# Two heads of q and k transposed side by side, and stacked by copies inside SBUF

## The chip, the cores and the metric

The kernel runs on one core of a Trainium2 chip. The metric is the device time of one execution in microseconds (us).

## What is computed

The reference runs attention over 8 batches and 8 heads of 576 positions by 64 dimensions, with all scores that lie more than tau under their row's maximum dropped, then two mixing layers. Only the attention is touched here:

```python
scores = scale * np.matmul(q, k.transpose(0, 1, 3, 2))
thresh = np.max(scores, axis=-1, keepdims=True) - tau
scores = np.where(scores >= thresh, scores, -1000000000.0)
scores = scores - np.max(scores, axis=-1, keepdims=True)
attn = np.exp(scores)
attn = attn / (np.sum(attn, axis=-1, keepdims=True) + 1e-09)
return np.matmul(attn, v).astype(np.float32)
```

## The kernel before

The attention walks over 32 pairs of heads. The 2 x 576 query rows of a pair are nine tiles of 128 rows: tiles 0 to 7 take the first 512 rows of the two heads in turn, tile 8 the last 64 rows of both. Every engine has its own list of steps for a pair, written out by hand: `PE_PLAN`, `ACT_PLAN` and `DVE_PLAN`. A step's name is its kind and number, and a trailing minus marks a step that belongs to the pair before. `scores` is the product q k^T of a tile in two halves of 288 keys (L434), `max` and `mask` are VectorE's row maximum (L561) and threshold product (L566), `exp` is ScalarE's small threshold operation and its exponential (L504, L506), `probs` and `rem` are transposes of the result (L395) with ScalarE's copy out of PSUM (L487), `pv` is the product with v (L476). `k`, `q` and `kq` prepare the next pair: transposes of its keys, its queries and its last 64 rows, with ScalarE's copies (L487, L491).

PSUM has three slots for scores, so tile i + 3 waits for the mask of tile i, and two banks `aux_ps` that all transposes and the product with v take in turn. So a group on TensorE waits until ScalarE has copied the group two before it.

The products are made in two passes of a rounded type: k is parted into k_hi and k_lo and q into a high and a low part, and one matmul multiplies the stack [q_hi; q_lo] on 128 partitions with [k; k], each head's 64 rows twice. Before, the doubling of k is done by the loads: `k_nat` holds each row twice side by side, so that its transpose has it on both halves of the partitions. q is parted in its natural layout by GpSimd (`q_split`, L318 and L320) and the two parts are transposed together. A pair thus takes 8 transposes for k, 8 for q and 2 for the last rows. After ScalarE's copy GpSimd parts k (`split_k`, L331 to L337). The first pair's k is parted by VectorE (L581 to L587).

SyncE (SP) issues the DMAs in the order of its `run`: `spread` (the reciprocal row sums to DRAM, L253 and L255, a wait for their landing, and their broadcast back, L258), the loads of q and k for the pair after the next (L202, L206, L235, L237), v, a chunk of weights (L241), and the store of x (L247). Between the runs of pairs 0 and 1 it issues seven small loads of the mixing's vectors (L289). ScalarE issues four large copies of weights from DRAM to DRAM, one after each of the exponentials 0 to 3 of pair 0 (L510). GpSimd's `run` also parts the chunk of weights (L343, L345) and multiplies x by the reciprocals (L358, L361).

## Time and profile before

| what | value |
|---|---|
| median of 3 runs | 1361.78 us (1361.44 to 1362.06) |
| the profiled execution, its own time | 1362.08 us |
| its span | 1360.3 us |
| busy TensorE, VectorE, ScalarE, GpSimd | 1325.3, 893.7, 876.1, 322.5 us |
| attention | from the start to about 629 us |

The span is what the trace covers; the time has 1.8 us more around it. Start times in the rows below count from the span's start. PE is TensorE's matmuls and PEld its weight loads, of which each matmul has one; PEld's starts are the better clock for TensorE's pace, since the ends of matmuls are modelled. DVE is VectorE, ACT ScalarE, POOL GpSimd, SPq SyncE's DMA queue. A bracket at the end of a row is idle time of the engine before it and what ended it.

### The profile page before, as it was taken

Reading aid. Unit: us, or ns where it says so; the run is one execution under the profiler, and the core shown is the slowest. Engines: PE = TensorE matmul, PEld = TensorE weight load, DVE = VectorE, ACT = ScalarE, POOL = GpSimd, SP = SyncE. Lnnn points to the kernel's source line nnn. Section 1 sums busy time; section 2 is a strip of 40 time slices with the busy share of each in tenths; the row PEclk is TensorE's granted clock in tenths of the full one; section 3 lists DMA queues with packets and bytes.
Section 4 is the critical chain, followed back from the end, with each engine's and each line's share of the span. In section 5 each row is a group of like instructions: output and inputs, shape, how many; then the busy total and the mean of one; then the engine's idle time right before and its main releaser. Section 6 shows DMA issues by size and latency. Waiting matters only on the chain.

```text
span 1360.3 us, 30705 instructions
## 1 busy us (share of the span) xinstructions
PE 1325.3 (97%) x9628; PEld 1161.0 (85%) x9628; DVE 893.7 (66%) x1969; ACT 876.1 (64%) x2086; POOL 322.5 (24%) x433
## 2 busy tenths in 40 slices
PE   6999999999999999996999999999999999999998
PEld 5777777777777777774999999999999999999997
DVE  4777777777777777775766765576647665756544
ACT  5888888888888888884545544554445445534432
POOL 3455554455544555533000000000000000000000
PEclk8999999999999999997999999999999999999999
DMA  8534433334333344322010011001110111011000
GB/s 234 131 101 113 116 94 105 104 103 116 101 103 104 99 115 116 93 77 87 19 34 17 18 34 42 19 18 34 34 40 5 34 34 34 1 42 34 17 9 32
DMA packets 141082, 90.49 MB, mean 67 GB/s; under 512 B 96192, under 2 KB 125120, under 8 KB 140992
## 3 DMA queue, kind: packets, MB, share of 16 engines
q1 hardware_dynamic: 137360, 82.47, 21.6%
q10 hardware_dynamic: 3632, 6.88, 1.5%
q8 instruction: 49, 0.80, 0.3%
q14 instruction: 41, 0.34, 0.1%
HBM read 70.29 MB, written 25.31 MB: 70 GB/s over the span
## 4 chain that ended last, share of the span: by engine, by line
PE 52%; DVE 1%; ACT 0%; issue 0%; DVEq 0%
PE kv_ps L805 15%; PE kv_ps L886 15%; PE vr_ps L805 15%; PE y_ps L870 7%; DVE mixed L998 0%; DVE xm_lo L1004 0%; ACT mixed L918 0%; DVE x L1057 0%; ACT xm_hi L926 0%; ACT y L935 0%; DVE square L1015 0%; DVE g_lo L1030 0%; DVE x_lo L1062 0%; DVE gated L1025 0%; ACT g_hi L966 0%
## 5 line engine op out<-in xcount | busy, mean ns | idle before, releaser
L566 DVE SCALAR_TENSOR_TENSOR probs<-score_ps,threshold,probs 128x576 f32<-128x576 f32 x288 | 234.5, 816 | 72.2 <-ACT probs L506 70.4
L561 DVE TENSOR_REDUCE neg_max<-score_ps 128x1 f32<-128x576 f32 x288 | 209.8, 747 | 95.6 <-PE score_ps L434 93.3
L506 ACT ACTIVATE probs<-score_ps,neg_max 128x576 f32<-128x576 f32 x288 | 215.3, 747 | 0.0
L487 ACT ACTIVATE probsT<-aux_ps 128x512 f32<-128x512 f32 x288 | 168.2, 615 | 44.3 <-PE aux_ps L395 44.3
L395 PE MATMUL aux_ps<-ident,probs 128*128 128x128 f32 x1280 | 190.5, 279 | 3.9 <-ACT k_raw L487 2.6
L434 PE MATMUL score_ps<-k_lo,qT 128*128 128x288 f32 x512 | 166.5, 340 | 5.0 <-DVE probs L566 4.2
L805 PE MATMUL kv_ps<-xm_hi,w_lo 128*128 128x288 f32 x512 | 152.5, 298 | 13.9 <-DVE xm_lo L1004 11.1
L395 PEld LDWEIGHTS aux_ps<-ident,probs 128*128 128x128 f32 x1280 | 144.5, 141 | 24.8 <-ACT probsT L487 10.9
L805 PE MATMUL kv_ps<-xm_hi,w_hi 128*128 128x288 f32 x512 | 152.5, 298 | 0.0
L805 PE MATMUL kv_ps<-xm_lo,w_hi 128*128 128x288 f32 x512 | 152.3, 297 | 0.0
L886 PE MATMUL kv_ps<-kk_hi,w_hi 128*128 128x288 f32 x512 | 151.1, 295 | 0.0
L886 PE MATMUL kv_ps<-kk_lo,w_hi 128*128 128x288 f32 x512 | 150.9, 295 | 0.0
L886 PE MATMUL kv_ps<-kk_hi,w_lo 128*128 128x288 f32 x512 | 150.2, 293 | 0.0
L434 PE MATMUL score_ps<-k_hi,qT 128*128 128x288 f32 x512 | 144.5, 297 | 0.0
L1070 DVE SCALAR_TENSOR_TENSOR gate<-x,taps,gate 128x288 f32<-128x288 f32 x256 | 132.2, 516 | 18.7 <-ACT gate L955 15.3
L476 PE MATMUL aux_ps<-probsT,v_nat 128*64 128x320 f32 (+1 forms) x1024 | 138.3, 412 | 1.0 <-ACT probsT_rem L487 0.8
L795 POOL MEMSET x_in<- 128x4 f32 x7 | 0.7, 105 | 545.1 <-DVE mixed L998 545.1
L434 PEld LDWEIGHTS score_ps<-k_lo,qT 128*128 128x128 f32 x512 | 97.1, 190 | 21.3 <-issue 14.6
L805 PEld LDWEIGHTS kv_ps<-xm_hi,w_lo 128*128 128x128 f32 x512 | 97.6, 191 | 16.0 <-DVE xm_lo L1004 12.7
L476 PEld LDWEIGHTS aux_ps<-probsT,v_nat 128*64 128x64 f32 x1024 | 68.2, 136 | 49.8 <-issue 10.8
L955 ACT ACTIVATE gate<-x,taps 128x288 f32<-128x288 f32 x64 | 34.1, 533 | 115.4 <-DVE x L1057 115.4
L945 ACT ACTIVATE relu<-kv_ps 128x288 f32<-128x288 f32 x128 | 52.3, 409 | 86.0 <-PE kv_ps L805 83.6
(99 smaller groups left out, 3216.7 us busy)
## 6 DMA issues: line engine op xcount, KB each, us to landing
k_nat<-in_k SPq DMA_DIRECT2D x128, 128.0 KB, 2.5
recip_rows<-recip_scratch SPq DMA_DIRECT2D x64, 144.0 KB, 3.1
x_scratch<-x_out SPq DMA_DIRECT2D x32, 288.0 KB, 2.6
out<-y SPq DMA_DIRECT2D x36, 256.0 KB, 2.0
q_nat<-in_q SPq DMA_DIRECT2D x31, 256.0 KB, 2.8
v_nat<-in_v SPq DMA_DIRECT2D x31, 256.0 KB, 2.7
w_stage<-packed SPq DMA_DIRECT2D x32, 192.0 KB, 2.5
x_in<-x_scratch SPq DMA_DIRECT2D x8, 578.0 KB, 4.1
```

The costliest lines, as they stand in the source:

```text
L395: return nc.tensor.transpose(out, in_, ident[:])
L434: last = nc.tensor.matmul(score_ps[i % SLOTS][:, half, 0:HALF], w, m, start=(term == 0), stop=(term == len(parts) - 1))
L476: last = nc.tensor.matmul(bank[D * h:D * (h + 1), 0:cols.stop - cols.start], v_nat[rows, cc % 2, h * FULL + t if t < FULL else MIX, :], m, ...
L487: return nc.scalar.activation(out, in_, ACT.Copy)
L506: nc.scalar.activation(tile_halves(i), scored(i), ACT.Exp, bias=neg_max[:, i:i + 1], scale=1.0).then_inc(exp_done, 1)
L561: nc.vector.tensor_reduce(neg_max[:, i:i + 1], scored(i), mybir.AxisListType.XY, ALU.max, negate=True).then_inc(max_ready, 1)
L566: nc.vector.scalar_tensor_tensor(tile_halves(i), scored(i), threshold[:, i:i + 1], tile_halves(i), ALU.is_ge, ALU.mult, accum_out=row_sum[ ...
L805: last = nc.tensor.matmul(ps, w, m, start=(n == 0), stop=(n == 3 * len(terms) - 1))
L870: last = nc.tensor.matmul(y_ps[i % 2][:], g[:, ch, col:col + P], w[:, ch, :], start=(n == 0), stop=(n == 3 * C - 1))
L886: last = nc.tensor.matmul(kv_ps[u][:, 0:HT], w, m[:, j, :], start=(n == 0), stop=(n == 3 * CF - 1))
L945: nc.scalar.activation(relu[:, i % 2, :], kv_ps[i % 4][:, 0:HT], ACT.Relu).then_inc(relu_done, 1)
L1070: nc.vector.scalar_tensor_tensor(gate[:, u, :], x2[:, u, t:t + HT], taps[:, t, u:u + 1], gate[:, u, :], ALU.mult, ALU.add).then_inc(conv_s ...
```

## The change

q and k of the pair's two heads are loaded side by side in the columns of `qk_nat`, each once, so that one transpose of 128 by 128 gives head 0 on partitions 0 to 63 and head 1 on 64 to 127. The last rows of q and k lie in `rem_nat` and take one transpose. A pair has 4 + 4 + 1 transposes in three groups in place of 18 in five. ScalarE copies the results to `q_raw` and `k_raw`. GpSimd now parts both after the transposes: `split_k` as two rounding copies and two subtractions over 640 and 576 columns, and after it `split_q` as two rounding copies and one subtraction over 640 columns. Each part then lies on the wrong half of the partitions for one of its uses, and SyncE copies it over within SBUF: `stack_k` waits for the whole of `split_k` and issues four DMAs of 64 partitions by 576 or 640 columns, `stack_q` waits for `split_q` and issues two of 64 by 640. TensorE's `scores0` of a pair waits for all six.

In the plans the preparing steps of the next pair are moved from the end of a pair to its start, and `exp8`, `max8`, `mask8` and `probs3` from the next pair to the end of their own. In SyncE's `run` the loads of q and k come first, then `stack_k`, `spread`, `stack_q` and the rest. In GpSimd's `run` the two splits come ahead of the weights' chunk. At the start SyncE stacks pair 0 as well, and the 12 warming matmuls of 512 columns are 14 of 128 columns in another type. The diff's core:

```diff
--- before.py
+++ after.py
 PE_PLAN = steps("""
-    scores0 probs3- probs7- scores1 pv0- scores2 probs6- probs8- scores3 q0 rem1- scores4
-    probs0 pv1- kq0 scores5 k0 rem0 scores6 probs2 k1 scores7 probs1 q1 scores8 probs4 probs5
+    scores0 k0 q0 scores1 probs7- probs6- scores2 kq0 pv0- probs8- scores3 probs0 rem1- scores4
+    scores5 pv1- scores6 probs3 probs4 scores7 rem0 probs2 scores8 probs5 probs1
 """)
 ACT_PLAN = steps("""
-    probs3- exp8- probs7- exp0 exp1 pv0- probs6- probs8- q0 rem1- probs0 exp2 exp3 exp4 pv1-
-    kq0 k0 rem0 exp5 probs2 k1 exp6 probs1 q1 exp7 probs4 probs5
+    k0 q0 probs7- probs6- exp0 kq0 exp1 exp2 pv0- probs8- probs0 rem1- exp3 exp4 exp5 pv1-
+    probs3 probs4 exp6 rem0 probs2 exp7 probs5 probs1 exp8
 """)
 DVE_PLAN = steps("""
-    max8- max0 max1 mask8- mask0 mask1 recip0- max2 max4 max3 mask2 mask3 max5 mask4 max6
-    mask5 max7 mask6 mask7
+    max0 recip0- max1 max2 mask0 mask1 mask2 max3 max4 max5 mask3 mask4 max6 mask5 max7 mask6
+    max8 mask7 mask8
 """)
-FIRST_PREPARE = steps("k0 kq0 k1 q0 q1")
+FIRST_PREPARE = steps("k0 kq0 q0")
...
-        q_nat = sb("q_nat", [P, 2, TILES, D])
-        k_nat = sb("k_nat", [P, 2, TILES, 2, D])
+        qk_nat = sb("qk_nat", [P, 2, 2, FULL, 2 * D])
+        rem_nat = sb("rem_nat", [P, 2, 2 * D])
         v_nat = sb("v_nat", [P, 2, TILES, D])
-        q_split = sb("q_split", [P, TILES, 2, D])
-        qT = sb("qT", [P, 2, 2, MAIN], F32R)
-        q_rem = sb("q_rem", [P, 2, 4, REM], F32R)
-        k_raw = sb("k_raw", [P, 2 * S])
-        k_hi = sb("k_hi", [P, 2, 2 * S + REM], F32R)
-        k_lo = sb("k_lo", [P, 2, 2 * S + REM], F32R)
+        q_raw = sb("q_raw", [P, QW])
+        k_raw = sb("k_raw", [P, KW])
+        q_lo = sb("q_lo", [P, QW], F32R)
+        q_all = sb("q_all", [P, 2, 2 * QW + REM], F32R)
+        k_hi = sb("k_hi", [P, 2, S + KW], F32R)
+        k_lo = sb("k_lo", [P, 2, S + KW], F32R)
...
+        def load_qk(eng, n, name, it, c, loaded):
+            for h in range(2):
+                eng.dma_start(qk_nat[:, c % 2, n, :, h * D:(h + 1) * D],
+                              heads[name][it * 4 + (2 * c + h), 0:MAIN, :].rearrange(
+                                  "(p t) d -> p t d", t=FULL)).then_inc(loaded[c % 2], 16)
+            eng.dma_start(rem_nat[n * REM:(n + 1) * REM, c % 2, :].rearrange("p (h d) -> p h d", h=2),
+                          heads[name][bass.ds(it * 4 + 2 * c, 2), MAIN:S, :].rearrange(
+                              "h p d -> p h d")).then_inc(loaded[c % 2], 16)
...
-                def load_k(it, c):
-                    slot = c % 2
-                    for twice in range(2):
-                        for h in range(2):
-                            head = it * 4 + (2 * c + h)
-                            k_to = k_nat[:, slot, :, twice, :]
-                            sp.dma_start(k_to[:, h * FULL:(h + 1) * FULL, :], heads["k"][head, 0:MAIN, :].rearrange(
-                                "(p t) d -> p t d", t=FULL)).then_inc(k_loaded[slot], 16)
-                            sp.dma_start(k_to[REM * h:REM * (h + 1), MIX, :],
-                                         heads["k"][head, MAIN:S, :]).then_inc(k_loaded[slot], 16)
+                def stack_q(it, c):
+                    par = c % 2
+                    sp.wait_ge(q_steps, count(it, c, 3, 3))
+                    sp.dma_start(q_all[REM:P, par, 0:QW].bitcast(F32), q_lo[0:REM, :].bitcast(F32)).then_inc(q_stacked, 16)
+                    sp.dma_start(q_all[0:REM, par, H1:].bitcast(F32), q_lo[REM:P, :].bitcast(F32)).then_inc(q_stacked, 16)
+                def stack_k(it, c):
+                    sp.wait_ge(k_steps, count(it, c, 4, 4))
+                    for kk in (k_lo, k_hi):
+                        own = kk[:, c % 2, :].bitcast(F32)
+                        sp.dma_start(own[REM:P, 0:S], own[0:REM, 0:S]).then_inc(k_stacked, 16)
+                        sp.dma_start(own[0:REM, S:], own[REM:P, S:]).then_inc(k_stacked, 16)
...
                 def run(it, c):
+                    if c <= PAIRS - 3:
+                        sp.wait_ge(aux_full, turns(it, prepared(c - 1)))
+                        load_q(sp, it, c + 2)
+                        load_k(sp, it, c + 2)
+                    if c < PAIRS - 1:
+                        stack_k(it, c + 1)
                     if c > 0:
                         spread(it, c - 1)
-                    if c <= PAIRS - 3:
-                        sp.wait_ge(aux_full, turns(it, prepared(c - 1)))
-                        load_q(sp, it, c + 2)
-                        load_k(it, c + 2)
                     if c < PAIRS - 1:
+                        stack_q(it, c + 1)
                         if c > 0:
                             sp.wait_ge(aux_full, turns(it, number_of(c - 1, "pv", 1) + 1))
                         load_v(sp, it, c + 1)
...
-                load_k(0, 0)
+                load_k(sp, 0, 0)
                 load_q(sp, 0, 1)
-                load_k(0, 1)
+                load_k(sp, 0, 1)
+                stack_k(0, 0)
+                stack_q(0, 0)
                 run(0, 0)
...
-                def split_q(it, c):
-                    wait(q_loaded[c % 2], count_loaded(it, c, 3))
-                    nc.gpsimd.tensor_copy(q_split[:, :, 0, :].bitcast(F32R), q_nat[:, c % 2, :, :]).then_inc(q_steps, 1)
-                    wait(q_steps, count(it, c, 2, 1))
-                    nc.gpsimd.tensor_tensor(q_split[:, :, 1, :], q_nat[:, c % 2, :, :], q_split[:, :, 0, :],
+                def split_q(it, c, run):
+                    wait(aux_copied, turns(it, 1 + max(number(run, (x, 0, False)) for x in ("q", "kq"))))
+                    for at in (0, H1):
+                        nc.gpsimd.tensor_copy(q_all[:, c % 2, at:at + QW], q_raw[:]).then_inc(q_steps, 1)
+                    wait(q_steps, count(it, c, 3, 1))
+                    nc.gpsimd.tensor_tensor(q_lo[:], q_raw[:], q_all[:, c % 2, 0:QW].bitcast(F32),
                                             ALU.subtract).then_inc(q_steps, 1)
                 def split_k(it, c, run):
-                    for h in range(2):
-                        ready = max(number(run, ("k", h, False)), number(run, ("kq", 0, False)))
-                        wait(aux_copied, turns(it, ready + 1))
-                        to = slice(h * S, (h + 1) * S)
-                        hi, lo = k_hi[:, c % 2, :], k_lo[:, c % 2, :]
-                        if h == 1:
-                            nc.gpsimd.tensor_copy(hi[:, 2 * S:], k_raw[:, S:S + REM])
-                        nc.gpsimd.tensor_copy(hi[:, to], k_raw[:, to]).then_inc(k_steps, 1)
-                        wait(k_steps, count(it, c, 4, 2 * h + 1))
-                        if h == 1:
-                            nc.gpsimd.tensor_tensor(lo[:, 2 * S:], k_raw[:, S:S + REM], hi[:, 2 * S:].bitcast(F32),
-                                                    ALU.subtract)
-                        nc.gpsimd.tensor_tensor(lo[:, to], k_raw[:, to], hi[:, to].bitcast(F32),
+                    wait(aux_copied, turns(it, 1 + max(number(run, (x, 0, False)) for x in ("k", "kq"))))
+                    parts = ((slice(S, S + KW), k_raw[:]), (slice(0, S), k_raw[:, REM:]))
+                    for to, raw in parts:
+                        nc.gpsimd.tensor_copy(k_hi[:, c % 2, to], raw).then_inc(k_steps, 1)
+                    wait(k_steps, count(it, c, 4, 2))
+                    for to, raw in parts:
+                        nc.gpsimd.tensor_tensor(k_lo[:, c % 2, to], raw, k_hi[:, c % 2, to].bitcast(F32),
                                                 ALU.subtract).then_inc(k_steps, 1)
...
                 def run(it, c):
                     if c > 0:
                         sums(it, c - 1)
-                        split_w(it, c - 1)
                     if c < PAIRS - 1:
                         split_k(it, c + 1, c)
+                        split_q(it, c + 1, c)
                     if c > 0:
+                        split_w(it, c - 1)
                         normalize(it, c - 1)
-                    if c < PAIRS - 2:
-                        wait(aux_full, turns(it, prepared(c)))
-                        split_q(it, c + 2)
-                split_q(0, 0)
-                pool.wait_ge(aux_full, prepared(-1))
-                split_q(0, 1)
+                split_q(0, 0, -1)
...
-                pe.wait_ge(ident_made, 2)
-                for _ in range(12):
-                    nc.tensor.matmul(aux_ps[0][:], q_rem[:, 0, 0:2, :], q_rem[:], start=True, stop=True)
                 pe.wait_ge(ident_made, 3)
...
                             if i == 0:
-                                pe.wait_ge(aux_copied, turns(it, prepared(c - 1)))
-                                pe.wait_ge(k_steps, count(it, c, 4, 2))
-                            if i == 1:
-                                pe.wait_ge(k_steps, count(it, c, 4, 4))
+                                pe.wait_ge(q_stacked, count(it, c, 32, 32))
+                                pe.wait_ge(k_stacked, count(it, c, 64, 64))
...
                         elif kind == "k":
-                            pe.wait_ge(k_loaded[(c + 1) % 2], count_loaded(it, c + 1, 8))
+                            pe.wait_ge(k_loaded[(c + 1) % 2], count_loaded(it, c + 1, 3))
                             for t in range(FULL):
-                                last = transpose(blocks[:, t, :], k_nat[:, (c + 1) % 2, i * FULL + t, :, :])
+                                last = transpose(blocks[:, t, :], qk_nat[:, (c + 1) % 2, 1, t, :])
                         elif kind == "q":
-                            pe.wait_ge(q_steps, count(it, c + 1, 2, 2))
+                            pe.wait_ge(q_loaded[(c + 1) % 2], count_loaded(it, c + 1, 3))
                             for t in range(FULL):
-                                last = transpose(blocks[:, t, :], q_split[:, i * FULL + t, :, :])
+                                last = transpose(blocks[:, t, :], qk_nat[:, (c + 1) % 2, 0, t, :])
                         elif kind == "kq":
-                            pe.wait_ge(k_loaded[(c + 1) % 2], count_loaded(it, c + 1, 8))
-                            pe.wait_ge(q_steps, count(it, c + 1, 2, 2))
-                            transpose(blocks[:, 0, :], q_split[:, MIX, :, :])
-                            last = transpose(blocks[:, 1, :], k_nat[:, (c + 1) % 2, MIX, :, :])
+                            pe.wait_ge(k_loaded[(c + 1) % 2], count_loaded(it, c + 1, 3))
+                            pe.wait_ge(q_loaded[(c + 1) % 2], count_loaded(it, c + 1, 3))
+                            last = transpose(blocks[:, 0, :], rem_nat[:, (c + 1) % 2, :])
...
+                for _ in range(14):
+                    nc.tensor.matmul(aux_ps[0][:, 0:P], ident[:], ident[:], start=True, stop=True)
...
                         elif kind == "q":
-                            scale_q(qT[:, nxt, i, :], bank[:]).then_inc(aux_copied, 1)
+                            scale_q(q_raw[:, 2 * REM:], bank[:]).then_inc(aux_copied, 1)
                         elif kind == "k":
-                            copy(k_raw[:, i * (S + REM):i * (S + REM) + MAIN], bank[:]).then_inc(aux_copied, 1)
+                            copy(k_raw[:, REM:S], bank[:]).then_inc(aux_copied, 1)
                         elif kind == "kq":
-                            scale_q(q_rem[:, nxt, 0:4:3, :], blocks[:, 0, :].rearrange("p (h q) -> p h q", h=2))
-                            copy(k_raw[:, MAIN:S + REM], blocks[:, 1, :]).then_inc(aux_copied, 1)
+                            scale_q(q_raw[:, 0:REM], bank[:, 0:REM])
+                            copy(k_raw[:].rearrange("p (a b) -> p a b", b=REM)[:, 0:TILES + 1:TILES, :],
+                                 bank[:, REM:2 * REM].unsqueeze(1).broadcast_to([P, 2, REM])).then_inc(aux_copied, 1)
```

## Rows read from the trace of the kernel before

**Rows 1.** Windows: busy us and instructions of each engine, granted clock, DMA share, GB/s.

```profile
200.00:300.00 100.00, 99.84 (x766) 76.30 (x764) 72.79 (x150) 88.42 (x204) 55.09 (x73) 1.00 0.40 107
```

**Rows 2.** Timeline, PEld: first weight load of scores0 of pair 2 and of pair 31.

```profile
51.64 0.19 PEld L434 LDWEIGHTS score_ps<-k_lo,qT 128*128 128x128 f32 x1
...
594.52 0.19 PEld L434 LDWEIGHTS score_ps<-k_lo,qT 128*128 128x128 f32 x1
```

**Rows 3.** Timeline, PEld: a scores step, a group of four transposes, what follows.

```profile
269.99 0.19 PEld L434 LDWEIGHTS score_ps<-k_lo,qT 128*128 128x128 f32 x1
...
270.51 0.49 PEld L395 LDWEIGHTS aux_ps<-ident,k_nat 128*128 128x128 f32 x4
270.97 0.25 PEld L395 LDWEIGHTS aux_ps<-ident,probs 128*128 128x128 f32 x2
```

**Rows 4.** Timeline, ScalarE, in a steady pair.

```profile
270.30 0.37 ACT L491 ACTIVATE q_rem<-aux_ps,q_scale 128x128 fp32r<-128x128 f32 x1
270.57 0.27 ACT L487 ACTIVATE k_raw<-aux_ps 128x128 f32<-128x128 f32 x1
271.28 0.60 ACT L487 ACTIVATE k_raw<-aux_ps 128x512 f32<-128x512 f32 x1 [0.45 <-PE aux_ps L395]
...
273.80 0.32 ACT L504 ACTIVATE threshold<-neg_max,tau_down 128x1 f32<-128x1 f32 x1
...
274.60 0.63 ACT L487 ACTIVATE probsT<-aux_ps 128x512 f32<-128x512 f32 x1
275.08 0.73 ACT L491 ACTIVATE qT<-aux_ps,q_scale 128x512 fp32r<-128x512 f32 x1
```

**Rows 5.** Timeline, GpSimd: the first head's k is parted.

```profile
272.01 0.66 POOL L332 CAST k_hi<-k_raw 128x576 fp32r<-128x576 f32 x1 [6.60 <-ACT k_raw L487]
272.82 1.43 POOL L337 TENSOR_TENSOR k_lo<-k_raw,k_hi 128x576 fp32r<-128x576 f32 x1
```

**Rows 6.** Timeline, SyncE's DMA issues: spread, then loads.

```profile
266.27 0.70 SPq L253 DMA_DIRECT2D recip_scratch<-recip_T  x1
267.01 0.62 SPq L255 DMA_DIRECT2D recip_scratch<-recip_T  x1
268.65 1.14 SPq L258 DMA_DIRECT2D recip_rows<-recip_scratch  x2
270.07 0.40 SPq L202 DMA_DIRECT2D q_nat<-in_q  x1
...
273.42 0.58 SPq L235 DMA_DIRECT2D k_nat<-in_k  x1
274.10 0.57 SPq L237 DMA_DIRECT2D k_nat<-in_k  x1
```

**Rows 7.** DMA view, 100 to 500 us: KB of each, median us from issue to landing.

```profile
recip_rows<-recip_scratch SPq DMA_DIRECT2D x44, 144.0 KB, 3.1
x_scratch<-x_out SPq DMA_DIRECT2D x21, 288.0 KB, 2.6
```

**Rows 8.** DMA view, whole span.

```profile
out<-y SPq DMA_DIRECT2D x36, 256.0 KB, 2.0
```

**Rows 9.** DMA view, 14 to 45 us: loads beside the copies of weights.

```profile
k_nat<-in_k SPq DMA_DIRECT2D x4, 128.0 KB, 12.0
```

**Rows 10.** Timeline, the start: q_scale, the first split, pair 0's first scores.

```profile
7.10 0.14 DVE L553 TENSOR_SCALAR q_scale<-tau_sb 128x1 f32<-128x1 f32 x1
10.76 0.46 DVE L582 CAST k_hi<-k_raw 128x576 fp32r<-128x576 f32 x1 [3.52 <-ACT k_raw L487]
11.26 0.76 DVE L587 TENSOR_TENSOR k_lo<-k_raw,k_hi 128x576 fp32r<-128x576 f32 x1
...
14.01 0.40 PE L434 MATMUL score_ps<-k_lo,qT 128*128 128x288 f32 x1 [0.78 <-ACT qT L491]
```

**Rows 11.** Timeline, SyncE: first of the small loads, and the first issue behind them.

```profile
28.27 0.69 SPq L289 DMA_DIRECT2D mu<-in_moe_mu_k  x1
...
42.61 0.75 SPq L253 DMA_DIRECT2D recip_scratch<-recip_T  x1
```

More of the change, by code:

```diff
@@ L261, in run @@
                 def run(it, c):
-                    if c > 0:
-                        spread(it, c - 1)
                     if c <= PAIRS - 3:
@@ L395, in transpose, with query @@
                     return nc.tensor.transpose(out, in_, ident[:])
+                def query(h, i, par):
+                    at = h * (H1 - REM) + (0 if i == MIX else (2 + h) * REM + i // 2 * P)
+                    return q_all[:, par, at:at + P]
                 def transpose_mixed(out, in_):
@@ L415, in run @@
                             if i == 0:
-                                pe.wait_ge(aux_copied, turns(it, prepared(c - 1)))
-                                pe.wait_ge(k_steps, count(it, c, 4, 2))
-                            if i == 1:
-                                pe.wait_ge(k_steps, count(it, c, 4, 4))
+                                pe.wait_ge(q_stacked, count(it, c, 32, 32))
+                                pe.wait_ge(k_stacked, count(it, c, 64, 64))
                             if c > 0 or i >= SLOTS:
                                 pe.wait_ge(probs_ready, count(it, c, TILES, i + 1 - SLOTS))
+                            ps = score_ps[i % SLOTS]
+                            parts = (i % 2,) if i < MIX else (0, 1)
                             for half in range(2):
-                                def keys(kk, at):
-                                    return kk[:, par, at + half * HALF:at + (half + 1) * HALF]
-                                if i < MIX:
-                                    h, t = i % 2, i // 2
-                                    parts = [(qT[:, par, h, t * P:(t + 1) * P], keys(kk, h * S)) for kk in (k_lo, k_hi)]
-                                else:
-                                    parts = [(q_rem[:, par, 2 * h:2 * h + 2, :], keys(kk, h * (S + REM)))
-                                             for kk in (k_lo, k_hi) for h in range(2)]
-                                for term, (w, m) in enumerate(parts):
-                                    last = nc.tensor.matmul(score_ps[i % SLOTS][:, half, 0:HALF], w, m,
-                                                            start=(term == 0), stop=(term == len(parts) - 1))
+                                terms = [(kk, h) for kk in (k_lo, k_hi) for h in parts]
+                                for n, (kk, h) in enumerate(terms):
+                                    at = S * h + (REM if h and i == MIX else 0) + half * HALF
+                                    last = nc.tensor.matmul(ps[:, half, 0:HALF], query(h, i, par), kk[:, par, at:at + HALF],
+                                                            start=(n == 0), stop=(n == len(terms) - 1))
                             last.then_inc(scores_full, 1)
@@ L572, in run @@
                             nc.vector.reciprocal(recip[:], row_sum[:, cc % 2, :]).then_inc(recip_ready, 1)
[L574 to L587 removed]
+                dve.wait_ge(aux_copied, 1 + max(number(-1, (x, 0, False)) for x in ("k", "kq")))
+                parts = ((slice(S, S + KW), k_raw[:]), (slice(0, S), k_raw[:, REM:]))
+                for to, raw in parts:
+                    nc.vector.tensor_copy(k_hi[:, 0, to], raw).then_inc(k_steps, 1)
+                dve.wait_ge(k_steps, 2)
+                for to, raw in parts:
+                    nc.vector.tensor_tensor(k_lo[:, 0, to], raw, k_hi[:, 0, to].bitcast(F32),
                                             ALU.subtract).then_inc(k_steps, 1)
```

31 lines of the change are left out of this document (13 added, 18 removed).

## The prediction, made before the changed kernel was seen to run

> **What bounds the kernel now.** I read the windows view first. In the middle of the attention TensorE is busy for 99.84 of 100 us, ScalarE for 88.42, VectorE for 72.79 and GpSimd for 55.09, at a granted clock of 1.00 [rows 1]. The reader should see an engine with no room beside one with little. Next the pace: scores0 of pair 2 starts at 51.64 and that of pair 31 at 594.52, so a pair takes 542.88 / 29 = 18.72 us [rows 2]. Weight loads show what a step costs on TensorE: a scores step of four matmuls runs from 269.99 to 270.51, 0.52 us, and four transposes from 270.51 to 270.97, 0.46 us, so 0.115 each [rows 3]. TensorE's order of work bounds the attention, with short waits for the two banks that ScalarE empties. The mixing after it is untouched.
>
> **What is removed.** Nine of 18 transposes of a pair: 9 x 0.115 = 1.04 us of TensorE, 1.0 rounded down. ScalarE loses one copy for k and one for q, starts 0.48 and some 0.58 apart (a copy of 512 columns starts at 274.60 and the next step at 275.08; the scaling one lasts 0.10 longer) [rows 4]: 1.06 us. Both bounds thus fall by the same amount, and a pair bound as before would take 18.72 - 1.0 = 17.7 us. Over 29 pairs that is 29 us. VectorE's work per pair is the same. k's loads fall from eight DMAs to three, and q's stay at three.
>
> **What is added: a loop through four engines.** The old stacking cost nothing after GpSimd. Now scores0 of the next pair waits for k and q of that pair to be transposed, copied, parted and stacked, and these steps only begin behind scores0 of this pair. What is queued behind the wait on TensorE is the whole next pair, its preparing transposes included, so a late stack delays its own successor and the loop's length becomes the pace. I add it up from scores0 at 0, with ScalarE free, as it is if TensorE has waited.
>
> - TensorE: scores0 to 0.52, k0 to 0.98. ScalarE starts a copy 0.77 after the first of four transposes (270.51 to 271.28) [rows 3, 4], so k0's copy is at 1.29 and q0's at 1.77 to 2.35. probs6- needs the bank of q0, so it starts at 2.5 and its copy is at 3.25 to 3.75. exp0 takes 0.80 (273.80 to 274.60), to 4.55, and kq0's two copies about 0.27 each by the old ones of 0.37 and 0.27 at 270.30 and 270.57 [rows 4]. Sum: 5.1 us. (Without a wait before, ScalarE is some 0.35 later.)
> - GpSimd starts 0.13 after the copy's end (271.28 + 0.60 to 272.01) [rows 4, 5]. The casts take 0.66 us for 576 columns and the subtraction 1.43, 0.15 behind the cast [rows 5]. For 640 columns I scale by 1.11: 0.73 and 1.59. split_k is 0.13 + 0.73 + 0.66 + 0.15 + 1.59 + 1.43, less about 0.2 for starts that overlap: 4.5 us. k is ready at 9.6. split_q follows with 0.73 + 0.73 + 1.59, less 0.1: 2.95, at 12.5.
> - SyncE: stack_k issues four DMAs. Issues in a row start 0.74 apart in spread's stores (266.27 and 267.01), 0.67 apart in k's loads, and two broadcasts end 1.14 after the first's start, under 0.6 each. The least duration is 0.40, of one after a pause [rows 6]. No row shows a copy from SBUF to SBUF. I take 0.62 each, since these run back to back, and 0.40 to 0.70 as bounds: 2.5 us (1.6 to 2.8).
> - spread stands between stack_k and stack_q. It runs from 266.27 to the next issue at 270.07, 3.8 us, of which 1.0 is the wait for the two stores to land [rows 6]. Its input is there by then, since rem1- is copied at about 9. The bound below is 3.8, above 4.4 if the stores queue behind 600 KB of stacks.
> - stack_q: its second DMA starts 0.62 later and lands after 2.0 us (256 KB, alone on the queue) [rows 8] to 3.1 (144 KB broadcast from DRAM) [rows 7]. The store of x takes 2.6. The copies are 160 KB and read SBUF in long rows, so I take 2.3, nearest to the 2.0.
>
> The sum is 5.1 + 4.5 + 2.5 + 3.8 + 0.6 + 2.3 = 18.8 us, and with all SyncE terms at their ends 5.1 + 4.5 + 1.6 + 3.8 + 0.4 + 2.0 = 17.4 and 5.1 + 4.5 + 2.8 + 4.4 + 0.7 + 3.1 = 20.6. It is over the 17.7 of TensorE's work. So TensorE waits 1.1 us at every scores0, and the pace is 18.8 in place of 18.72: 29 x 0.08 = +2 us. split_q at 12.5 is not late; SyncE comes to it at 15.9.
>
> The Trainium skill ("DMA: Bandwidth & Descriptors", Anatomy of one DMA) gives a fit of 2.0 us and bytes over 436 GB/s for a DMA on GpSimd's path. By that an estimate for 160 KB is 2.4 us, and the sum above would be 18.9. Its rules for kernel authors say that two transfers to disjoint partition halves aren't worth splitting since they share the same engines, which speaks against halves as the unit here; no row before shows it.
>
> **Once only: the start.** Before, pair 0's scores start at 14.01. ScalarE can't scale before q_scale at 7.24 [rows 10]. From there: k0 and kq0 copied at 8.4, VectorE's parts of k (0.46 and 0.76 for 576 columns [rows 10], twice, the larger ones a tenth more) to 11.1, q's copy at 9.5 and GpSimd's part of it to 12.6, stack_k to 13.6, stack_q's last issue at 14.2, landed at 16.5, scores0 about 16.6: +2.6 us.
>
> Then SyncE's seven small loads cost 42.61 - 28.27 = 14.3 us of issue [rows 11], and they stand ahead of stack_k and stack_q of pair 2. Before, nothing urgent stood behind them. Pair 0's scores at 16.6, kq0 and GpSimd's two splits for pair 1 (5.0 and 7.5) to 29.1, stack_q to 30.3, v and weights 2.5, small loads from 32.8 to 47.1, six loads 3.7, stack_k 2.5, spread 3.8, stack_q and landing 2.9: pair 2's scores0 at 60.0, against 51.64 [rows 2], +8.4 us. Pair 1's stacks fall beside the copies of weights, where a load took 12.0 us to land [rows 9], and SyncE's issues may be held up there as well. That can add up to 4, and I take 1.6, so +10 us in all (6 to 13), the first 2.6 included. If the 14.3 us were not in the way, +3 would be left. The tail has one group of four transposes less: -0.5.
>
> **Sum.** 1362.08 (the profiled execution's own time, 1360.3 of it span) + 10 + 2 - 0.5 = 1373.6, 1373.3 beside the median, which is 0.3 lower. The two one-time terms are rough; I state 1373.
>
> **Rivals.**
> - The stacks are hidden. If an issue costs 0.40 and the landing 2.0, the loop is 17.4, under 17.7; TensorE's work sets the pace, -29 + 9.5 = 1342. For it: the short issues of 0.40 exist [rows 6]. Against: DMAs issued in a row take 0.57 to 0.74 each there. Chance 0.14.
> - The loop binds, but just: issues 0.55, landing 2.0, so 5.1 + 4.5 + 2.2 + 3.8 + 0.55 + 2.0 = 18.15, 29 x -0.57 + 9.5 = 1355. Chance 0.16. It decides at 18.72 - 9.5 / 29 = 18.39 us: shorter loops make the kernel faster, longer ones slower.
> - The loop is longer: spread's stores and the last stacks queue behind the four stacks. Spread 4.3, issues 0.67, landing 2.6 give 5.1 + 4.5 + 2.7 + 4.3 + 0.7 + 2.6 = 19.9, 29 x 1.18 + 9.5 = 1406; half of that excess, 19.35, gives 1390. Chance 0.2 for 19.2 and more.
> - The start costs little (SyncE's small loads go faster away from the copies of weights): pace 18.8, start +3: 1366. Chance 0.08.
>
> **How the numbers follow.** The forecast, loops of 18.4 to 19.2 with the start near +10, has 0.42 and its own range is 1361 to 1385. A measurement of this kernel can tell about 0.2% from no change, 2.7 us. Faster takes the first two rivals, 0.14 and 0.13 of 0.16, and nothing else: 0.27. Within 0.2% takes 0.03 of the second, 0.03 of the last and the forecast's lower edge, 0.07: 0.13. The rest is slower: 0.60. For 8 in 10 I leave out most of the first rival and the far end of the third: 1346 to 1394.
>
> **What the profile would show.** TensorE should have an idle of about 1 us before the first weight load of each pair's scores0, released by a DMA into q_all, and busy under 96% in the window of rows 1. kq0's copies should end about 5.1 behind scores0, GpSimd's k_lo 4.5 later, SyncE's four stacks start 0.6 apart, spread take 3.8, and the last stack land 2.3 after its issue. Pair 2's scores0 should start near 61, with an idle of several us. I am wrong if TensorE has no idle there and a pair takes 17.7, or if ScalarE or VectorE hold the new order up.

## The result and the profile after

The changed kernel takes 1419.5 us (median; 1419.0 to 1423.2) against 1361.9 in the same session: a ratio of 1.043, with an interval of 1.041 to 1.0446. The span went from 1360.3 to 1421.3. The forecast of 1373 and its range up to 1394 are missed on the slow side. The profiled execution of the changed kernel is the slowest of the four, 1423.2 us. Times below are medians; of the run with `spread` ahead of both stacks one execution of four (1409.6 us) fell in a slower state and is left out. The lines below answer to [rows 1] and [rows 2]; the first two are the page's busy times and the windows view (its stretch and length, then busy us and instructions of PE, PEld, DVE, ACT, POOL, then granted clock, DMA share, GB/s).

```profile
PE 1308.0 (92%) x9356; PEld 1154.6 (81%) x9356; DVE 900.4 (63%) x1967; ACT 841.0 (59%) x2022; POOL 338.9 (24%) x404
...
200.00:300.00 100.00, 87.93 (x649) 67.88 (x648) 67.32 (x138) 74.82 (x175) 49.12 (x59) 0.97 0.50 131
```

```profile
17.56 0.28 PEld L449 LDWEIGHTS score_ps<-k_lo,q_all 128*128 128x128 f32 x1 [8.83 <-DMA q_all<-q_lo]
...
62.37 0.19 PEld L449 LDWEIGHTS score_ps<-k_lo,q_all 128*128 128x128 f32 x1 [4.15 <-issue]
...
659.89 0.19 PEld L449 LDWEIGHTS score_ps<-k_lo,q_all 128*128 128x128 f32 x1 [2.19 <-DMA q_all<-q_lo]
```

No engine is full any more: TensorE fell from 99.84 to 87.93 busy, and ScalarE, VectorE and GpSimd fell as well. A pair takes (659.89 - 62.37) / 29 = 20.60 us against 18.72. The waits view of 100 to 500 us names who is waited for (us in all, times, longest; a mean of 38.4 / 17 = 2.3):

```profile
PE score_ps L449 <- DMA q_all<-q_lo: 38.4, 17, 2.9
```

The span's 61.0 us divide so. Pair 2's scores start at 62.37 in place of 51.64: +10.7. Then 29 x 1.88 = +54.6. What is left is -4.4, and it lies in the mixing, from its first matmul to the end: 724.5 us (1421.3 - 696.84) against 728.8 (1360.3 - 631.46). From the last pair's scores0 to that matmul it is 36.95 and 36.94, the same. The mixing's code is untouched. The first 60 weight loads of the mixing take 14.3 us before and 10.0 after, which is all of the difference. These rows, of before and then of after, show what stands beside them:

```profile
631.76 0.61 POOL L787 CAST w_out_hi<-y 128x512 fp32r<-128x512 f32 x1 [2.55 <-DMA y<-in_moe_w_out]
632.60 1.52 DVE L998 SCALAR_TENSOR_TENSOR mixed<-x_in,mu,mixed 128x288 f32<-128x288 f32 x1
634.05 0.86 DVE L1004 TENSOR_TENSOR xm_lo<-mixed,xm_hi 128x288 fp32r<-128x288 f32 x1
634.96 0.29 PEld L805 LDWEIGHTS kv_ps<-xm_hi,w_lo 128*128 128x128 f32 x1 [1.49 <-DVE xm_lo L1004]
```

```profile
697.56 0.51 DVE L1008 SCALAR_TENSOR_TENSOR mixed<-x_in,mu,mixed 128x288 f32<-128x288 f32 x1
697.99 0.45 DVE L1014 TENSOR_TENSOR xm_lo<-mixed,xm_hi 128x288 fp32r<-128x288 f32 x1
699.05 0.65 POOL L797 CAST w_out_hi<-y 128x512 fp32r<-128x512 f32 x1 [4.46 <-DMA y<-in_moe_w_out]
```

VectorE's same two operations take 0.51 and 0.45 us while GpSimd is idle, and 1.52 and 0.86 while GpSimd parts w_out. Before, GpSimd begins 0.3 us after the mixing's first matmul (631.76), so TensorE waits for VectorE three times, 3.1 us in all, and its clock is at the lower level for the first 10.4 us; after, GpSimd begins 2.2 us behind it (699.05), those waits are gone, and it is so for 4.4 us. The experiments below bear this out: in the two with fillers GpSimd begins 0.0 and 0.4 us behind, and the mixing takes 729.0 and 729.1 us; in the other seven it begins 1.6 to 2.3 behind, and the mixing takes 724.4 to 725.4. Moving GpSimd's work by itself was not tried.

**One pair, step by step.** The timeline of after, with PEld, ScalarE's last copy (kq0 for k), GpSimd's two splits and SyncE's issues:

```profile
271.39 0.19 PEld L449 LDWEIGHTS score_ps<-k_lo,q_all 128*128 128x128 f32 x1 [2.16 <-issue]
...
276.07 0.28 ACT L503 ACTIVATE k_raw<-aux_ps 128x128 f32<-128x128 f32 x1
...
276.49 1.33 POOL L359 CAST k_hi<-k_raw 128x640 fp32r<-128x640 f32 x2 [4.15 <-ACT k_raw L503]
277.97 2.93 POOL L362 TENSOR_TENSOR k_lo<-k_raw,k_hi 128x640 fp32r<-128x640 f32 x2 [0.15 <-POOL k_hi L359]
...
280.93 0.53 SPq L260 DMA_DIRECT2D k_lo<-k_lo  x1
281.50 0.60 SPq L261 DMA_DIRECT2D k_lo<-k_lo  x1
282.14 0.60 SPq L260 DMA_DIRECT2D k_hi<-k_hi  x1
282.79 0.60 SPq L261 DMA_DIRECT2D k_hi<-k_hi  x1
283.51 0.69 SPq L276 DMA_DIRECT2D recip_scratch<-recip_T  x1
284.24 0.61 SPq L278 DMA_DIRECT2D recip_scratch<-recip_T  x1
285.86 1.14 SPq L281 DMA_DIRECT2D recip_rows<-recip_scratch  x2
287.13 0.51 SPq L252 DMA_DIRECT2D q_all<-q_lo  x1
287.68 0.60 SPq L253 DMA_DIRECT2D q_all<-q_lo  x1
...
291.56 0.25 PEld L449 LDWEIGHTS score_ps<-k_lo,q_all 128*128 128x128 f32 x1 [2.80 <-DVE probs L582]
...
297.81 0.29 ACT L503 ACTIVATE k_raw<-aux_ps 128x128 f32<-128x128 f32 x1
```

Read it as a loop. kq0 is copied 4.96 us after scores0 (276.35). GpSimd ends 4.55 later, SyncE starts 0.03 after that, its issues run for 6.75 to the last one, and scores0 follows 3.88 behind: 20.17 in all. The bracket of the next scores0 names a release by VectorE, but its product for probs was long done. The DMA is what came last.

The last row shows a second thing. In the pair that starts at 291.56, kq0 is copied after 6.54 us. TensorE waits 2.2 to 2.8 us at scores0 (once 3.1), and in every second or third pair the granted clock is at its lower level (1.2 GHz) behind the wait. Eight transposes show it: 0.92 us of weight loads in the one pair, 1.71 in the other.

```profile
271.89 0.92 PEld L412 LDWEIGHTS aux_ps<-ident,qk_nat 128*128 128x128 f32 x8
...
292.45 1.71 PEld L412 LDWEIGHTS aux_ps<-ident,qk_nat 128*128 128x128 f32 x8
```

The DMA view of 100 to 500 us (KB each, median us from issue to landing) has the disputed transfer:

```profile
q_all<-q_lo SPq DMA_DIRECT2D x40, 160.0 KB, 3.3
...
recip_rows<-recip_scratch SPq DMA_DIRECT2D x38, 144.0 KB, 3.1
...
k_hi<-k_hi SPq DMA_DIRECT2D x19, 160.0 KB, 2.6
```

The same 160 KB copy lands in 2.6 us as part of k's stack and in 3.3 as part of q's, behind the two broadcasts. The four stacks of k are themselves issued 0.6 apart, so the later ones have up to three copies of 144 to 160 KB under way ahead of them, and they land no later for it.

**The start.** Pair 1's scores0, and SyncE's small loads:

```profile
39.30 0.29 PEld L449 LDWEIGHTS score_ps<-k_lo,q_all 128*128 128x128 f32 x1 [4.61 <-issue]
...
30.86 0.60 SPq L253 DMA_DIRECT2D q_all<-q_lo  x1
...
34.14 0.53 SPq L317 DMA_DIRECT2D mu<-in_moe_mu_k  x1
...
45.88 1.25 SPq L218 DMA_DIRECT2D qk_nat<-in_q  x2
```

Pair 1 starts 8.4 us behind its last copy's issue (30.86 to 39.30), since that copy, beside ScalarE's copies of weights, takes 8.2 us to land. The small loads hold SyncE from 34.14 to 45.88.

### The profile page after: what moved, and what is told of

It is laid out like the page before. It is cut to its first block, busy times and chain, and to the rows that moved or that the text cites. A ratio compares the mean times of both kernels' runs of the same rounds, so it can differ in the third digit from the quotient of the medians.

```text
span 1421.3 us, 29572 instructions
## 1 busy us (share of the span) xinstructions
PE 1308.0 (92%) x9356; PEld 1154.6 (81%) x9356; DVE 900.4 (63%) x1967; ACT 841.0 (59%) x2022; POOL 338.9 (24%) x404
## 4 chain that ended last, share of the span: by engine, by line
PE 49%; DVE 1%; ACT 0%; issue 0%; DVEq 0%
PE kv_ps L896 14%; PE vr_ps L815 14%; PE kv_ps L815 13%; PE y_ps L880 7%; DVE xm_lo L1014 0%; DVE square L1025 0%; DVE mixed L1008 0%; ACT mixed L928 0%; DVE x L1067 0%; DVE kk_lo L1029 0%; ACT xm_hi L936 0%; ACT y L945 0%; DVE g_lo L1040 0%; DVE x_lo L1072 0%; DVE gated L1035 0%
## 5 line engine op out<-in xcount | busy, mean ns | idle before, releaser
L577 DVE TENSOR_REDUCE neg_max<-score_ps 128x1 f32<-128x576 f32 x288 | 215.0, 756 | 168.9 <-PE score_ps L449 164.9
L449 PE MATMUL score_ps<-k_lo,q_all 128*128 128x288 f32 x640 | 202.9, 346 | 86.6 <-DMA q_all<-q_lo 70.4
L449 PEld LDWEIGHTS score_ps<-k_lo,q_all 128*128 128x128 f32 x640 | 123.7, 200 | 110.0 <-issue 62.5
L503 ACT ACTIVATE probsT<-aux_ps 128x512 f32<-128x512 f32 x288 | 163.7, 604 | 55.6 <-PE aux_ps L412 52.0
L412 PE MATMUL aux_ps<-ident,probs 128*128 128x128 f32 x1280 | 184.1, 280 | 1.0 <-ACT probsT L503 0.8
L449 PE MATMUL score_ps<-k_hi,q_all 128*128 128x288 f32 x640 | 178.7, 307 | 0.0
L412 PEld LDWEIGHTS aux_ps<-ident,probs 128*128 128x128 f32 x1280 | 149.8, 143 | 22.6 <-issue 12.9
L449 PEld LDWEIGHTS score_ps<-k_hi,q_all 128*128 128x128 f32 x640 | 125.2, 201 | 0.0
```

Source lines behind the costliest of these rows:

```text
L412: return nc.tensor.transpose(out, in_, ident[:])
L449: last = nc.tensor.matmul(ps[:, half, 0:HALF], query(h, i, par), kk[:, par, at:at + HALF], start=(n == 0), stop=(n == len(terms) - 1))
L503: return nc.scalar.activation(out, in_, ACT.Copy)
L577: nc.vector.tensor_reduce(neg_max[:, i:i + 1], scored(i), mybir.AxisListType.XY, ALU.max, negate=True).then_inc(max_ready, 1)
```

## The experiments

The theory, A: the pace is the loop through ScalarE, GpSimd and SyncE, and what makes it long is SyncE's order, `spread` ahead of `stack_q`, by the time it takes and by what it leaves in the queue. Against it stood: the issues themselves, whatever their order; the clock, which falls in the wait; the start's small loads; the bytes or the repeated row of the broadcasts.

**q's stack ahead of spread.**

```diff
                         stack_k(it, c + 1)
+                        stack_q(it, c + 1)
                     if c > 0:
                         spread(it, c - 1)
                     if c < PAIRS - 1:
-                        stack_q(it, c + 1)
```

> The changed kernel with stack_q moved ahead of spread in SyncE's order, all else as it is. Theory A (the loop through GpSimd and SyncE sets the pace, since the stacks of q are issued behind spread): k is ready 9.55 us after scores0 and q 12.4, so the last stack is issued at 13.0 and lands by 15.6 to 16.6; that is under the 17.7 of TensorE's work, the wait at scores0 goes, the granted clock stays at 1.00 and a pair takes 17.7 in place of 20.6 us. Time 1419.5 - 29 x 2.9 - 3 = 1332 (1325 to 1345). Within it, A1 (the last stack lands late because it queues behind the two broadcasts of spread): issue to landing 2.5 us in place of 3.3. A2 (a copy within SBUF of this shape takes 3.3 us by itself): it stays 3.3. Rival B (the new order of steps on ScalarE and VectorE is itself slower, the wait only covers it): a pair still takes 18.5 us or more, time 1358 or more.

Measured: 1339.8 us, ratio 0.984 (0.9827 to 0.9859), faster than before the change, and within what theory A gave (1325 to 1345). Windows, DMA view, and two weight loads of scores0, those of pairs 2 and 15:

```profile
200.00:300.00 100.00, 98.95 (x759) 75.50 (x758) 74.79 (x159) 87.12 (x206) 57.91 (x67) 1.00 0.56 148
```

```profile
q_all<-q_lo SPq DMA_DIRECT2D x46, 160.0 KB, 2.6
```

```profile
57.66 0.19 PEld L449 LDWEIGHTS score_ps<-k_lo,q_all 128*128 128x128 f32 x1
...
290.25 0.19 PEld L449 LDWEIGHTS score_ps<-k_lo,q_all 128*128 128x128 f32 x1
```

That is (290.25 - 57.66) / 13 = 17.89 us per pair, and TensorE is full again. The copy lands in 2.6, near A1's 2.5, and its last issue stands 4.4 us ahead of scores0, so it is no longer what is waited for. The pace is TensorE's own work, 17.7 by the prediction's count of transposes. The whole gain of the transposes was there, and one line in SyncE's order had it hidden. The start costs 6.0 us of it.

**spread ahead of both stacks.** This tells the time that spread takes on the path from its place directly ahead of q.

```diff
-                    if c < PAIRS - 1:
-                        stack_k(it, c + 1)
                     if c > 0:
                         spread(it, c - 1)
                     if c < PAIRS - 1:
+                        stack_k(it, c + 1)
                         stack_q(it, c + 1)
```

> The changed kernel with spread moved ahead of stack_k and stack_q, as it stood before the change, all else as it is. Spread's input is there 9.0 us after scores0, it takes 3.8, stack_k 2.6, stack_q's last issue is at 16.0. A1 (queueing behind the broadcasts made the landing late; here they are 4 us away): landing 2.5, a pair 18.6 us, time about 1419.5 - 29 x 2.0 = 1361 (1355 to 1375). A2 (the copy takes 3.3 to 3.6 by itself): a pair 19.6 or more, and with the clock falling in some pairs about 20: 1390 to 1405. Rival B: no change, since the order of the copies is not what binds: 1419.

Measured: 1393.6 us (1386.9 to 1399.9), ratio 1.0217 (1.0187 to 1.0246); a pair takes 19.0 to 19.8 us at the full clock, and the clock falls in 8 of 28. DMA view and SyncE's last broadcasts and last q issue ahead of a scores0:

```profile
q_all<-q_lo SPq DMA_DIRECT2D x40, 160.0 KB, 3.3
...
k_hi<-k_hi SPq DMA_DIRECT2D x20, 160.0 KB, 3.3
```

```profile
275.41 1.14 SPq L281 DMA_DIRECT2D recip_rows<-recip_scratch  x2
...
279.80 0.60 SPq L253 DMA_DIRECT2D q_all<-q_lo  x1
...
283.84 0.19 PEld L448 LDWEIGHTS score_ps<-k_lo,q_all 128*128 128x128 f32 x1 [2.43 <-issue]
```

A1's number, 1361, was missed, and the time lies in the range of A2, by which the copy takes 3.3 to 3.6 by itself. The run before rules A2 out as the cause: there the copy lands in 2.6. What was wrong is A1's premise that 4 us of distance are enough. k's stacks now stand directly behind the broadcasts and land late, 3.3 in place of 2.6, and q's, issued 0.6 apart behind them, as late: the delay is passed on. In the mean pair this order brought 0.7 us (19.9 in place of 20.6).

**Short rows in spread.** The same issues and waits, with 4 KB in place of 144; the rest of `recip_rows` is zeroed once.

```diff
-                        sp.dma_start(recip_rows[D * h:D * (h + 1), :],
-                                     rows[h].partition_broadcast(D)).then_inc(rows_loaded, 16)
+                        sp.dma_start(recip_rows[D * h:D * (h + 1), 0:16],
+                                     rows[h, 0:16].partition_broadcast(D)).then_inc(rows_loaded, 16)
...
+                nc.gpsimd.memset(recip_rows[:], 0.0)
```

> The changed kernel with the two broadcasts of spread cut to 16 of 576 columns (64 B in place of 2304 B per row); their number, their issue and the wait ahead of them stay, and most of x is multiplied by zero. A1 (the stacks of q land late since the broadcasts ahead of them in the queue are slow to move): issue to landing of the copies into q_all 2.6 us as in the run with stack_q ahead of spread, in place of 3.3; a pair shorter by 0.7 to 1.0 and the clock falls less often, 1419.5 - 29 x (0.7 to 1.5) = 1376 to 1399. A2 (the late landing has to do with the number of DMAs in a row, not with their bytes): 3.3 and 1419.

Measured: 1380.0 us, ratio 1.0134 (1.0117 to 1.0151), within A1's range.

```profile
q_all<-q_lo SPq DMA_DIRECT2D x42, 160.0 KB, 2.6
...
recip_rows<-recip_scratch SPq DMA_DIRECT2D x42, 4.0 KB, 2.3
```

```profile
270.84 0.19 PEld L450 LDWEIGHTS score_ps<-k_lo,q_all 128*128 128x128 f32 x1 [1.82 <-DVE probs L583]
```

A pair takes 4.97 + 4.57 + 0.03 + 6.72 + 2.85 = 19.14 us, and all of them from pair 2 on 19.1 to 19.2. The copy of q lands in 2.6 without the bytes ahead of it. The wait is 1.6 to 1.9 us, and the clock stays at 1.00 from pair 2 to the last. This is nearly the loop that was forecast, 18.8.

**Other rows of the same size.** Is it the bytes, or 64 reads of one row of DRAM?

```diff
                         sp.dma_start(recip_rows[D * h:D * (h + 1), :],
-                                     rows[h].partition_broadcast(D)).then_inc(rows_loaded, 16)
+                                     heads["v"][h].rearrange("(p t) d -> p (t d)", t=TILES)).then_inc(rows_loaded, 16)
```

> The changed kernel with the two broadcasts of spread replaced by loads of the same size and number (64 rows of 2304 B each) that read 64 different rows of v in place of one row 64 times; x is multiplied by values of v. Is it the bytes that make the stacks behind them late, or the repeated reading of one DRAM row? If the bytes: issue to landing of the copies into q_all stays 3.3 us, a pair 20.6, time 1415 to 1423. If the repeated row: 2.6 to 2.8 as with the short rows, a pair 19.1 to 19.4, time 1375 to 1390.

Measured: 1414.1 us, ratio 1.038 (1.0359 to 1.0404).

```profile
q_all<-q_lo SPq DMA_DIRECT2D x38, 160.0 KB, 3.0
...
recip_rows<-in_v SPq DMA_DIRECT2D x38, 144.0 KB, 2.8
```

Of the 0.7 us more than in the run with short rows, distinct rows leave 0.4. So the size of the loads ahead is the larger part, and the repeated row adds 0.3. Neither expectation had a landing of 3.0, and the time, just under the range for the bytes, says less than it seems: the pairs at full clock became 0.3 us shorter (19.6 in place of 19.9), but with waits of 1.9 to 2.5 us the clock still fell in 13 of 28 pairs, as many as in the changed kernel. The bytes alone can't be all either: the stacks of k carry as many ahead of each other and land in 2.6. What differs is that they copy within SBUF, while the broadcasts and these loads read DRAM; which part of that counts was not tried.

**Fillers for the clock.** Matmuls of 128 columns ahead of the wait keep TensorE at work; 16 of them, and then 8.

```diff
                             if i == 0:
+                                if c > 0:
+                                    g = number(c, next(x for x in plan if x[0] in GROUPS))
+                                    pe.wait_ge(aux_copied, turns(it, g - 1))
+                                    for _ in range(8):
+                                        nc.tensor.matmul(aux_ps[g % 2][:, 0:P], ident[:], ident[:], start=True, stop=True)
                                 pe.wait_ge(q_stacked, count(it, c, 32, 32))
```

> The changed kernel with 16 matmuls of 128 columns on the identity (1.8 us at full clock) put on TensorE ahead of the wait of scores0; their results are overwritten. It keeps TensorE at work while it would wait. Theory C (in every second or third pair the granted clock falls to the lower of its two levels after the wait, which makes the preparing transposes late by 1.55 us and lengthens the loop): clock near 1.00, every pair about 19.9 us, time 1419.5 - 29 x 0.7 = 1399 (1392 to 1404). Rival: the clock is a by-product and costs nothing: 1417 to 1422. If the fillers themselves are in the way, slower than 1422.

Measured: 1450.9 us, ratio 1.066 (1.0646 to 1.0682), the third of its expectations: the fillers themselves are in the way. This one was badly sized. A filler takes two weight loads, so the 16 last 3.65 us and end after the stacks have landed. It says nothing on the clock's price.

```profile
272.28 3.65 PEld L442 LDWEIGHTS aux_ps<-ident 128*128 128x128 f32 x32 [0.51 <-ACT probsT L508]
```

> As the run with 16 filling matmuls, but with 8, since each of them turned out to take two passes, 0.23 us, so that 16 outlasted the wait they were to fill (3.65 us against some 2.2). Eight take 1.8 us and end before the stacks land. Theory C (the fall of the granted clock after the wait costs 1.55 us in every second or third pair, by slow transposes): clock at 1.00, kq0's copies 4.97 us behind scores0 in every pair, a pair 19.9 us in place of 20.6, time 1419.5 - 29 x 0.7 = 1399 (1392 to 1404). Rival: the clock costs nothing: 1417 to 1422.

Measured: 1408.6 us, ratio 1.034 (1.0323 to 1.0362).

```profile
279.10 1.86 PEld L442 LDWEIGHTS aux_ps<-ident 128*128 128x128 f32 x16 [0.51 <-ACT probsT L508]
...
281.75 0.19 PEld L454 LDWEIGHTS score_ps<-k_lo,q_all 128*128 128x128 f32 x1 [0.79 <-DVE probs L587]
```

```profile
200.00:300.00 100.00, 97.09 (x746) 75.72 (x745) 69.07 (x140) 76.16 (x180) 51.28 (x61) 1.00 0.51 130
```

Eight end before the stacks do and leave 0 to 0.8 us of wait, 0.3 on average; the row shows the longest. The clock is 1.00, kq0 is copied after 4.97 in every pair, and a pair takes 20.05 in place of 20.60. So the clock's price is 0.55 us per pair, 16 us in all, and the loop at full clock is the rest. The time fell by less, 10.9 us, and lies between theory C's range (1392 to 1404) and the rival's (1417 to 1422): 4.5 us went into the mixing, as told above, and the profiled execution of the changed kernel is 3.6 us slower than its median, so that at the median the price is nearer 0.4 (an estimate, 0.55 - 3.6 / 29). That the clock costs time is shown, its size is rough. The window also shows why a busy share alone is no proof: TensorE is 97% busy here, a good part of it with fillers.

**kq0 earlier.** If the loop is the pace, shortening it anywhere must help. kq0 moves right behind q0 in both plans, SyncE's order stays as in the change.

```diff
-    scores0 k0 q0 scores1 probs7- probs6- scores2 kq0 pv0- probs8- ...
+    scores0 k0 q0 kq0 scores1 probs7- probs6- scores2 pv0- probs8- ...
...
-    k0 q0 probs7- probs6- exp0 kq0 exp1 ...
+    k0 q0 kq0 probs7- probs6- exp0 exp1 ...
```

> The changed kernel with kq0 put right behind q0 in TensorE's and ScalarE's order (it stood behind scores2 and exp0), SyncE's order as in the change, with stack_q behind spread. Theory A (the pace is the sum of the loop's terms): kq0's copies end some 2.9 us behind scores0 in place of 4.97, so the loop is 2.9 + 4.6 + 6.7 + 3.6 = 17.8, about TensorE's own 17.8; the wait at scores0 nearly goes and with it the fall of the clock. A pair 17.8 to 18.3, time 1419.5 - 29 x 2.5 = 1347 (1337 to 1355). Rival B (the pace isn't the loop's sum): 1405 or more.

Measured: 1349.7 us, ratio 0.990 (0.9887 to 0.9919). Two neighbouring scores0:

```profile
279.21 0.19 PEld L449 LDWEIGHTS score_ps<-k_lo,q_all 128*128 128x128 f32 x1 [0.19 <-issue]
...
297.63 0.19 PEld L449 LDWEIGHTS score_ps<-k_lo,q_all 128*128 128x128 f32 x1 [0.56 <-issue]
```

kq0 is copied after 2.8 to 3.3 us in place of 4.97, and the mean pair takes 18.15. From pair 3 on TensorE waits 0.3 us on average, 0.65 at most, and its clock stays at 1.00. The landing is still 3.3. The loop is thus shown from its other end, on ScalarE: another order of TensorE's and ScalarE's steps shortens the path by 2 us, and the pace follows, down to 0.3 us above the pair with q's stack ahead of spread.

**The small loads.** The seven go behind SyncE's run of pair 30, alone and with q's stack ahead of spread.

```diff
-                for dst, src in small_loads:
-                    sp.dma_start(dst, src, allow_slow_non_contiguous=True).then_inc(small_loaded, 16)
                 run(0, 1)
...
                 run(0, PAIRS - 2)
+                for dst, src in small_loads:
+                    sp.dma_start(dst, src, allow_slow_non_contiguous=True).then_inc(small_loaded, 16)
```

> The changed kernel with the seven small loads moved from behind SyncE's run of pair 0 to behind that of pair 30, all else as it is. Theory D (the small loads stood in front of pair 2's stacks, but pair 1's own late start hides most of it): pair 2's scores0 at about 59 to 60 in place of 62.4, time 1419.5 - 3 = 1416.5, or up to 3 more if the late loads delay the end. The prediction's own reading (the loads cost the whole of what the start lost beyond 3 us): 1412.

Measured: 1420.8 us (1416.5 to 1423.1), ratio 1.043 (1.0407 to 1.0453). Pair 2's scores0 starts at 60.59 against 62.37, and nothing of this is left at the end. The prediction's statement that without them +3 would be left, on which its last rival rests, is refuted: of the +10.7 they hold 1.8. Behind them stands the other path: pair 1 starts at 39.3 in both kernels, 6 us later than before, and a round of the loop from there ends at about 60.

> The run with stack_q ahead of spread, with the seven small loads moved behind SyncE's run of pair 30 as well. With a pace that TensorE sets, pair 2 is no longer held by the small loads: its scores0 at 38.7 + 17.8 = 56.5 in place of 57.7, so 1 us less, and up to 2 us more if the late loads delay the last pairs: 1338 to 1341, against 1339.8 of stack_q first alone. If the small loads still held the start in some way that pair 1's late start hides, 1335.

Measured: 1338.8 us, ratio 0.9825 (0.9809 to 0.9841).

```profile
58.92 0.19 PEld L449 LDWEIGHTS score_ps<-k_lo,q_all 128*128 128x128 f32 x1
```

This can't be told from q's stack ahead of spread alone (0.9827 to 0.9859). The time is as expected, but not by its reason: pair 2's scores0 comes at 58.92, not 1 us earlier than 57.66 but 1.3 later. Pair 1 lasts 19.0 us in both runs, so the small loads hold nothing there; it starts later (39.92 for 38.69).

## Why the prediction was wrong, step by step

The mechanism was right: a loop through four engines that hides what TensorE has saved. Its length was the error.

- TensorE and ScalarE up to kq0's copy: 5.1 forecast, 4.97 measured. GpSimd: 4.5 and 4.56. SyncE's first issue: 0.03 behind, taken as nothing. ScalarE's part was added up from old rows ([rows 4]), GpSimd's scaled from them by the columns ([rows 5]), and both held.
- SyncE's issues from first to last: 2.5 + 3.8 + 0.6 = 6.9 forecast, 6.72 measured. The four stacks start 0.6 apart.
- **The landing is the step that failed.** It was put at 2.3, near the store of 256 KB alone on its queue [rows 8]; it is 3.3 at the median of both copies, and scores0 comes 3.6 to 3.7 behind the last issue on average. Two causes in it are told apart. With no DRAM load just ahead such a copy takes 2.6, so 0.3 was my choice of row. The other 0.7 is the queue: the two broadcasts issued just ahead, with 288 KB, are still under way. The run with short rows takes it away, and the one with other rows of the same size gives 0.4 of it back. The bound of 3.1 was also too low. The prediction named this wait in its third rival, but only for the stacks of k as what is ahead, and gave it a chance of 0.2; the stacks turned out to add nothing. The broadcasts, which its own order put directly ahead of q, it charged with their issue alone. The loop at full clock comes to 4.97 + 4.56 + 0.03 + 6.72 + 3.6 = 19.9, to the digit that rival's 19.9, but by luck: its spread of 4.3 isn't there (283.51 to 287.13 is 3.6).
- **The clock wasn't in the sum at all.** With 1.1 us of wait foreseen it would have stayed up, as the run with short rows shows for 1.6 to 1.9. At 2.2 to 2.8 it falls in 13 of 28 pairs, and that adds 0.4 to 0.7: from 19.9 to 20.6. An error of one step thus set off a second. That 20.6 is also the upper end of the prediction's own sum is luck: that end is made of slower issues, a longer spread and a landing of 3.1, and has no clock in it.
- What was removed: 17.7 was forecast for TensorE's own work. With q's stack ahead of spread a pair takes 17.86, so this stands within 0.2.
- The start: +10 forecast, +10.7 measured, first scores0 at 17.56 for 16.6 and pair 2's at 62.37 for about 61. SyncE's steps from pair 1's stacks over the small loads to pair 2 went nearly as added up. What failed is the reading that without them +3 would be left. They hold 1.8, since pair 1, whose last copy takes 8.2 us to land beside the copies of weights, comes 6 us late by itself.
- The tail: -0.5 forecast for the attention's last pair, 0.0 measured. The mixing's -4.4 wasn't foreseen; it goes with the moment at which GpSimd parts w_out beside VectorE.

From 1373.6: the pace 20.6 in place of 18.8 makes 29 x 1.8 = +52, the start +0.7, tail and mixing -3.9, which is 1422.6 beside the span's 1421.3 + 1.8 = 1423.1.

The Trainium skill ("DMA: Bandwidth & Descriptors", Anatomy of one DMA) would have given 2.4 for the landing as an estimate, for another issuing engine; the measured 2.6 of the undisturbed copy is near it, and the 3.3 is not. The same page (Queues, rings and completion order) says that each of the 16 engines takes its queue's descriptors in order, and that a DMA's semaphore increment lands only after all earlier writes of that engine. The measured 2.6 behind 4 KB and 3.3 behind 144 KB loads agree with this. It does not tell which transfers ahead cost time: those of k's stacks don't.

## What to carry to other kernels

When a step is moved from an engine with free time onto a path that is waited for, write the path down as a loop and add up every DMA on it with what is issued ahead in the same queue: a landing time taken from a row holds only for what stood ahead of the transfer in that row. Here loads from DRAM just ahead added 0.4 to 0.7 us, and copies within SBUF nothing. Where the loop comes out near the bound, put the transfers that are waited for ahead of those that aren't; here this order was the difference between 4.3% slower and 1.6% faster. And price the clock as well where a wait on TensorE grows long: here it never fell with waits of up to 2.0 us in a pair, and did in about every second pair with waits of 2.1 and more.

## What the runs showed of the hardware

- A copy of 160 KB from SBUF to SBUF (64 partitions) lands 2.6 us after its issue, also with up to three such copies issued 0.6 us apart ahead of it. It lands after 3.3 behind two broadcasts of 144 KB on the same queue, and after 3.0 behind loads of that size from distinct rows. Four more copies between it and the broadcasts do not take the delay away.
- A broadcast of one row to 64 partitions lands in 3.1 us, a load of 64 distinct rows of that size in 2.8.
- With waits of 1.6 to 1.9 us per pair of 19.1 the granted clock stayed at 1.00. With waits of 2.2 to 2.8 per pair of 20.6 it fell to the lower level in every second or third pair. Between them, with 1.6 to 2.6 per pair of 19.9, it fell in 8 of 28 pairs, each time behind a wait of 2.1 or more.
- In the mixing, VectorE's operations on 128x288 take 0.45 to 0.52 us with GpSimd idle, and 0.86 to 1.5 beside GpSimd's casts and subtractions.
- A plain matmul in f32 on 128 columns takes two weight loads, 0.114 us each (3.65 / 32), a transpose of the same size one, 0.115 (0.92 / 8). So a filler costs 0.23 us.
